# Queries and keys of the first head pair in two transfers each, and a scaling in two pieces

## The chip, the cores and the metric

The kernel runs on one core of a Trainium2 chip. The core's engines run their own instruction streams and meet at semaphores: TensorE (matrix products), VectorE, ScalarE, GpSimd, and SyncE (SP), which here only starts transfers. 16 DMA engines move data between DRAM and the on-chip memory; a transfer is started by an engine's queue, and it raises a semaphore by 16 when it has landed. The metric is the device time of one execution in microseconds, lower is better.

## What is computed

Block-causal attention over 4 x 8 heads of 576 positions and 64 columns, then a dense feed-forward layer, then a layer that sends each token to one of 8 experts:

```python
scores = scale * np.matmul(q, k.transpose(0, 1, 3, 2))      # (4, 8, 576, 64), scale = 1/8
scores = np.where(block_i >= block_j, scores, -1000000000.0)  # blocks of 64 positions
attn = np.exp(scores - np.max(scores, axis=-1, keepdims=True))
attn = attn / (np.sum(attn, axis=-1, keepdims=True) + 1e-09)
x = np.matmul(attn, v)                                       # then (2304, 512)
h = x @ w_in
x = np.maximum(0.01 * h, h) @ w_out                          # 512 -> 2048 -> 512
# tokens with x @ w_skip > 0: x + gate_w * (relu(x @ w1[e]) @ w2[e]), e the best of 8 experts
```

## The kernel before

The span has three stages: attention for 16 pairs of heads (with the first product of the dense layer filled in between, from pair 5 on), the rest of the dense layer, and the experts. Only the first microseconds of the first stage concern the change.

**A pair of heads** lies in tiles of 128 partitions, one head in each half: `q_sb[p % 2]` and `k_sb[p % 2]`, 576 columns of four bytes each, for pair p. The products of a pair are cut into nine units. Eight are query tiles of 128 rows, four per head, and query tile qt needs only the keys up to column 128 (qt + 1). The ninth, unit `TAIL` = 4, holds the last 64 query rows of both heads and needs all 576 columns of the keys. For the first six pairs TensorE computes the scores in five groups (`scores_of_both`, whose number is n): group 0 is query tile 0 of both heads (columns 0 to 127), group 1 is query tile 1 (queries 128 to 255, keys 0 to 255), group 2 is unit 4 (the last 64 queries, all keys), groups 3 and 4 are query tiles 2 and 3. Group 2 also needs room in the score buffers, that is two finished exponentials.

**Order.** Each engine's order is written out by hand in a loop over steps s, one unit each. VectorE first scales the queries by 1/8 (`scale_q`, L1118, waiting for queries and keys on `s_qk`), then takes each unit's row maximum (`maximum`, L1140, in step s for unit s), and copies transposed probabilities (L1146). ScalarE takes the exponential (L977) in step s once the maximum is there. TensorE runs groups 0 and 1 as soon as `s_q` says that the queries are scaled, then transposes the probabilities of unit 0 (L1491), then group 2 (L1435). The scaling of pair 1's queries is VectorE's in step 4.

**Loads at the start.** SP's queue starts the queries of pair 0 (`load_q(e, 0)`, L576), then queries and keys of pair 1, then a small weight tile; ScalarE's queue starts the keys of pair 0 (`load_k(e, 0)`, L581) and two transfers of values. Both queues feed the same 16 DMA engines. A tile of 128 rows of 2304 bytes goes as 128 packets. GpSimd meanwhile builds constants and masks (L763 to L800); its instructions L783 to L790 work on 4 x 512 mask tiles.

Of the kernel before, what the change touches and what calls it, by code (L numbers as in the profile page):

```python
# [11 lines left out]
ALU = mybir.AluOpType  # L12
# [3 lines left out]
P = 128  # L16
B, H, S, D = 4, 8, 576, 64
# [19 lines left out]
TAIL = 4  # L37
ROW_PAIRS = 6
ROW_UNITS = ROW_PAIRS * UNITS
FIRST_SPLIT = 2 * ROW_PAIRS  # L40


# [110 lines left out]
def by_act(p):  # L153

    return (7, 8) if p < ROW_PAIRS else (3, 8)
# [48 lines left out]
def build(nc, q_t, k_t, v_r, w_in, w_out, w_gs, w1, w2, out):  # L204
    ctx = ExitStack()
    with ctx:
        def sb(name, shape, dt=F32, scope=ctx):
            return scope.enter_context(nc.sbuf_tensor(name, shape, dt))
# [4 lines left out]
        def sem(name):  # L213
            return ctx.enter_context(nc.semaphore(name))
# [27 lines left out]
        q_sb = [sb(f"q_sb{i}", [P, S], F32, r2) for i in range(2)]  # L242
        k_sb = [sb(f"k_sb{i}", [P, S], F32, r2) for i in range(2)]
# [121 lines left out]
        s_wg = sem("s_wg")  # L365
        s_qk = [sem(f"s_qk{i}") for i in range(2)]
        s_v = [sem(f"s_v{i}") for i in range(2)]
        s_q = sem("s_q")
        s_mask = sem("s_mask")
        s_maskd = sem("s_maskd")  # L370
# [92 lines left out]
        def s_slot(u):  # L463
            p, i = divmod(u, UNITS)
            return 10 * p + i + (i > TAIL)

        def s_freed(u):

            last = s_slot(u) + (u % UNITS == TAIL) - S_RING
            if last < 0:  # L470
                return 0
            p, c = divmod(last, 10)
            return UNITS * p + c + 1 - (c > TAIL)
# [94 lines left out]
        def pair_in(x, p):  # L568

            b, h = p // KC, 2 * (p % KC)  # L570
            return x[b, h:h + 2, :, :].rearrange("h d s -> (h d) s")

        def load_q(e, p):
            if p >= 2:
                e.wait_ge(s_score, UNITS * (p - 1))
            e.dma_start(q_sb[p % 2][:, :], pair_in(q_t, p)).then_inc(s_qk[p % 2], 16)  # L576

        def load_k(e, p):
            if p >= 2:
                e.wait_ge(s_score, UNITS * (p - 1))  # L580
            e.dma_start(k_sb[p % 2][:, :], pair_in(k_t, p)).then_inc(s_qk[p % 2], 16)  # L581

        def load_head(e, n):

            p, odd = divmod(n, 2)
            b, h = p // KC, 2 * (p % KC) + odd
            if n >= FIRST_SPLIT + 2:
                e.wait_ge(s_qlo, n - FIRST_SPLIT - 1)
                e.wait_ge(s_klo, n - FIRST_SPLIT - 1)
            for half in (0, D):  # L590
                e.dma_start(k_raw[odd][half:half + D, :], k_t[b, h, :, :]).then_inc(s_head[odd], 16)
            cut = S - D
            to = QW - D if odd else cut
            for half in (0, D):
                if odd:
                    e.dma_start(q_raw[odd][half:half + D, 0:cut], q_t[b, h, :, 0:cut]).then_inc(s_head[odd], 16)
                    e.dma_start(q_raw[odd][half:half + D, to:QW], q_t[b, h, :, cut:S]).then_inc(s_head[odd], 16)
                else:
                    e.dma_start(q_raw[odd][half:half + D, 0:S], q_t[b, h, :, :]).then_inc(s_head[odd], 16)
# [12 lines left out]
        def _(e):  # L612
            def copy_k(n):
                e.wait_ge(s_khi, n - FIRST_SPLIT + 1)
                e.dma_start(k2[n % 2][0:D, :].bitcast(F32), k_st[n % 2][0:D, :].bitcast(F32)).then_inc(s_k2[n % 2], 16)
# [61 lines left out]
                    e.wait_ge(loaded, 16 * done)  # L677
                e.dma_start(dst, src).then_inc(loaded, 16)

            load_q(e, 0)  # L680
            load_q(e, 1)
            load_k(e, 1)
            e.dma_start(wg[:, :, :], w_gs).then_inc(s_wg, 16)
            for s in range(STEPS):
                p, i = divmod(s, UNITS)
# [74 lines left out]
        def _(e):  # L760
# [44 lines left out]
            def low_k(n):  # L805
                i, m = n % 2, n - FIRST_SPLIT
                e.wait_ge(*before[0])
                e.wait_ge(s_khi, m + 1)
                e.tensor_tensor(k_st[i][D:P, :], k_raw[i][D:P, :], k_st[i][D:P, :].bitcast(F32),
                                ALU.subtract).then_inc(s_klo, 1)  # L810
                before[0] = s_klo, m + 1
# [136 lines left out]
        def _(e):  # L948
            def high_q(n):
                odd, m = n % 2, n - FIRST_SPLIT  # L950
                e.wait_ge(s_head[odd], (96 if odd else 64) * (m // 2 + 1))
                if m < 2:
                    e.wait_ge(s_gap, N_GAP)
                else:
                    e.wait_ge(s_score, UNITS * (n // 2 - 1) + (UNITS if odd else TAIL + 1))
                e.activation(q_hi[odd][:, :], q_raw[odd][:, :], ACT.Copy, scale=D ** -0.5).then_inc(s_qhi, 1)
# [62 lines left out]
                for src, dst in pt_views(u):  # L1019
                    e.activation(dst, src, ACT.Copy).then_inc(s_pta, 1)  # L1020

            load_k(e, 0)
            load_v(e, 0)
            for s in range(STEPS):
                p, i = divmod(s, UNITS)
# [87 lines left out]

        @block.vector
        def _(e):
            def scale_q(p):
                e.wait_ge(s_qk[p % 2], 32 * (p // 2 + 1))
                e.tensor_scalar(q_sb[p % 2][:, :], q_sb[p % 2][:, :], D ** -0.5, None, ALU.mult).then_inc(s_q, 1)  # L1118
# [16 lines left out]
            def maximum(u):  # L1135
                src = score_out(u)
                e.wait_ge(s_score, u + 1)
                if u >= 4:
                    e.wait_ge(s_exp, u - 3)
                e.tensor_reduce(out=neg_max[:, u % 4:u % 4 + 1], in_=src, axis=AX.XY if u % UNITS == TAIL else AX.X,  # L1140
                                op=ALU.max, negate=True).then_inc(s_max, 1)
# [38 lines left out]
                e.tensor_tensor(g_lo[j % G_RING][:, :, :], g_raw[j % RAW_RING][:, :, :],  # L1180
                                g_hi[j % G_RING][:, :, :].bitcast(F32), ALU.subtract).then_inc(s_glo, 1)

            scale_q(0)
            for s in range(STEPS):
                p, i = divmod(s, UNITS)
                if s < N_UNITS:
                    maximum(s)
                if 3 <= s < N_UNITS + 3 and (s - 3) % UNITS not in by_act((s - 3) // UNITS):
                    copy_turned(s - 3)
                if i == 4 and p + 1 < ROW_PAIRS:  # L1190
                    scale_q(p + 1)
                if ROW_PAIRS <= p + 1 < N_PAIRS:
                    if i == 3:
                        high_k(2 * p + 2)
                    if i == 5:
                        low_q(2 * p + 2)
                    if i == 7:
                        high_k(2 * p + 3)
                if i == 0 and ROW_PAIRS <= p < N_PAIRS:
                    low_q(2 * p + 1)  # L1200
                if i == 0 and 1 <= p <= N_PAIRS:
                    invert(p - 1)
                if i == 2 and 1 <= p <= N_PAIRS:
                    copy_inverse(p - 1)
                if o_at(s):
                    copy_o(*o_at(s))
# [211 lines left out]
        def _(e):  # L1418
            def scores_of_both(n):

                p, d = divmod(n, GROUPS)
                u = UNITS * p + GROUP_LAST[d]
                if d == 0:
                    e.wait_ge(s_q, p + 1)
                if n == 0:
                    e.wait_ge(s_const, N_CONST)
                if s_freed(u):
                    e.wait_ge(s_exp, s_freed(u))
                c = 2 * BANK * (n % 2)
                q, k = q_sb[p % 2], k_sb[p % 2]  # L1430
                heads = (slice(0, D), slice(D, P))
                if GROUP_LAST[d] == TAIL:
                    for half in range(2):
                        for own in heads:
                            last = e.matmul(ps_s[own, c + BANK * half:c + BANK * half + S // 2], q[own, DM:S],  # L1435
                                            k[own, S // 2 * half:S // 2 * (half + 1)], start=True, stop=True)
                    last.then_inc(s_score, 1)
                    return
                qt = head_tile(u)[1]
                cols = P * (qt + 1)  # L1440
                for h, own in enumerate(heads):
                    e.matmul(ps_s[:, c + BANK * h:c + BANK * h + cols], q[own, P * qt:P * qt + P], k[own, 0:cols],  # L1442
                             start=True, stop=False)
                for h, own in enumerate(heads):
                    last = e.matmul(ps_s[:, c + BANK * h + cols - D:c + BANK * h + cols], mask_q[own, :], mask_k[own, :],  # L1445
                                    start=False, stop=True)
                last.then_inc(s_score, 2)

            def scores(u):

                p, i = divmod(u, UNITS)
                if i in (0, TAIL):
# [3 lines left out]
                    e.wait_ge(s_qlo, n - FIRST_SPLIT + 1)  # L1456
                if u == ROW_UNITS:
                    e.wait_ge(s_maskd, 32)
# [98 lines left out]
            for s in range(STEPS):  # L1557
                if ROW_UNITS <= s + 2 < N_UNITS:
                    scores(s + 2)
                if 2 <= s < N_UNITS + 2:  # L1560
                    transposes(s - 2)
                p, i = divmod(s, UNITS)
# [4 lines left out]
                if i in GROUP_AT:  # L1567
                    n = GROUPS * (p + (i > TAIL + 2)) + GROUP_AT[i]
# [228 lines left out]
```

## Time and profile before

| What | us |
|---|---|
| Median of 3 runs | 785.87 |
| The three runs | 784.16, 785.87, 787.03 |
| The profiled execution | 787.15 |
| its span, first to last instruction | 785.4 |
| TensorE busy | 761.7 |
| VectorE, ScalarE, GpSimd busy | 368.1, 303.3, 148.5 |

The page counts a busy engine from the first to the last moment of an instruction; its chain of waits leads back from the last instruction to what released it. "ACTq" and "SPq" are the queues that start transfers; times in the trace count from the span's start. A row with x2 stands for two instructions in a row.

### The profile page before, as it was taken

Reading aid. Unit: us, or ns where it says so; the run is one execution under the profiler, and the core shown is the slowest. Engines: PE = TensorE matmul, PEld = TensorE weight load, DVE = VectorE, ACT = ScalarE, POOL = GpSimd, SP = SyncE. Lnnn points to the kernel's source line nnn. Section 1 sums busy time; section 2 is a strip of 40 time slices with the busy share of each in tenths; the row PEclk is TensorE's granted clock in tenths of the full one; section 3 lists DMA queues with packets and bytes.
Section 4 is the critical chain, followed back from the end, with each engine's and each line's share of the span. In section 5 each row is a group of like instructions: output and inputs, shape, how many; then the busy total and the mean of one; then the engine's idle time right before and its main releaser. Section 6 shows DMA issues by size and latency. Waiting matters only on the chain.

```text
span 785.4 us, 13538 instructions
## 1 busy us (share of the span) xinstructions
PE 761.7 (97%) x4738; PEld 645.2 (82%) x4738; DVE 368.1 (47%) x771; ACT 303.3 (39%) x711; POOL 148.5 (19%) x193
## 2 busy tenths in 40 slices
PE   7999999999999998999999999999999999999997
PEld 3555888888888887999988888888878879999996
DVE  5667465533333554023355456465564342444644
ACT  4566565544344553234432223222121131333533
POOL 3226564221121331100020000000000031222222
PEclk9999999999999999999999999999999999999999
DMA  4334777554444541375666656556562037778730
GB/s 125 97 126 141 210 201 201 169 140 127 126 135 127 150 113 52 89 209 166 188 175 183 200 154 183 158 165 188 159 176 69 28 112 249 229 255 256 239 124 4
DMA packets 97671, 121.68 MB, mean 155 GB/s; under 512 B 14226, under 2 KB 60578, under 8 KB 97608
## 3 DMA queue, kind: packets, MB, share of 16 engines
q1 hardware_dynamic: 94776, 116.50, 50.6%
q0 software_dynamic: 2080, 3.77, 1.5%
q8 instruction: 36, 0.59, 0.3%
q10 hardware_dynamic: 752, 0.59, 0.2%
q14 instruction: 27, 0.22, 0.1%
HBM read 89.35 MB, written 31.57 MB: 154 GB/s over the span
## 4 chain that ended last, share of the span: by engine, by line
PE 91%; ACT 2%; issue 2%; DVE 1%; SPq 1%; DMA 1%; POOL 1%; DVEq 0%; POOLq 0%; ACTq 0%
PE ps_hid L1755 10%; PE ps_h L1535 9%; PE ps_x L1588 9%; PE ps_x L1590 8%; PE ps_x L1589 8%; PE ps_h L1537 8%; PE ps_h L1536 8%; PE ps_o L1517 6%; PE ps_t L1491 4%; PE ps_y L1767 3%; PE ps_y L1768 3%; PE ps_y L1766 3%; PE ps_s L1478 2%; PE ps_s L1442 1%; PE ps_s L1479 1%
## 5 line engine op out<-in xcount | busy, mean ns | idle before, releaser
L1535 PE MATMUL ps_h<-xh,win_h 128*128 128x384 f32 x384 | 136.4, 355 | 3.1 <-ACT act L989 2.4
L1537 PE MATMUL ps_h<-xh,win_l 128*128 128x384 f32 x384 | 128.7, 335 | 0.0
L1536 PE MATMUL ps_h<-xl,win_h 128*128 128x384 f32 x384 | 128.6, 335 | 0.0
L1588 PE MATMUL ps_x<-wout_h,g_hi 128*128 128x512 f32 x288 | 114.7, 398 | 0.0
L1590 PE MATMUL ps_x<-wout_h,g_lo 128*128 128x512 f32 x288 | 112.4, 390 | 0.0
L1589 PE MATMUL ps_x<-wout_l,g_hi 128*128 128x512 f32 x288 | 112.2, 389 | 0.0
L989 ACT ACTIVATE act<-ps_h 128x384 f32<-128x384 f32 x96 | 47.2, 492 | 155.7 <-PE ps_h L1537 155.7
L977 ACT ACTIVATE prob<-ps_s,neg_max 128x128 f32<-128x128 f32 (+3 forms) x144 | 78.8, 550 | 28.0 <-DVE neg_max L1140 27.4
L1146 DVE COPY pt<-ps_t 128x384 f32<-128x384 f32 (+4 forms) x113 | 48.4, 436 | 81.6 <-PE ps_t L1491 81.2
L1140 DVE TENSOR_REDUCE neg_max<-ps_s 128x1 f32<-128x128 f32 (+3 forms) x144 | 71.8, 504 | 30.4 <-PE ps_s L1445 15.2
L1755 PEld LDWEIGHTS ps_hid<-rows_t,w_sb 128*128 128x128 f32 x704 | 80.2, 192 | 1.7 <-issue 0.8
L1180 DVE TENSOR_TENSOR g_lo<-g_raw,g_hi 128x512 fp32r<-128x512 f32 x72 | 49.5, 688 | 67.2 <-ACT g_hi L999 66.8
L1755 PE MATMUL ps_hid<-rows_t,w_sb 128*128 128x128 f32 x704 | 80.5, 275 | 0.0
L1535 PEld LDWEIGHTS ps_h<-xh,win_h 128*128 128x128 f32 x384 | 72.1, 188 | 10.2 <-ACT act L989 5.1
L1536 PEld LDWEIGHTS ps_h<-xl,win_h 128*128 128x128 f32 x384 | 72.3, 188 | 0.0
L1537 PEld LDWEIGHTS ps_h<-xh,win_l 128*128 128x128 f32 x384 | 72.1, 188 | 0.0
L1588 PEld LDWEIGHTS ps_x<-wout_h,g_hi 128*128 128x128 f32 x288 | 54.1, 188 | 12.3 <-issue 2.0
L1590 PEld LDWEIGHTS ps_x<-wout_h,g_lo 128*128 128x128 f32 x288 | 54.1, 188 | 11.6
L1589 PEld LDWEIGHTS ps_x<-wout_l,g_hi 128*128 128x128 f32 x288 | 54.1, 188 | 10.4
L999 ACT ACTIVATE g_hi<-g_raw 128x512 fp32r<-128x512 f32 x72 | 43.8, 630 | 47.0 <-DVE g_raw L1175 31.1
L1491 PE MATMUL ps_t<-ident,prob 128*128 128x128 f32 x339 | 58.9, 278 | 1.4 <-issue 0.7
L1175 DVE SCALAR_TENSOR_TENSOR g_raw<-g_raw 128x512 f32<-128x512 f32 x72 | 49.2, 685 | 14.6 <-DMA g_raw<-hidden 14.3
(185 smaller groups left out, 1065.6 us busy)
## 6 DMA issues: line engine op xcount, KB each, us to landing
w_sb<-in_w SPq DMA_DIRECT2D x64, 512.0 KB, 5.3
hidden<-act SPq DMA_DIRECT2D x96, 192.0 KB, 2.3
g_raw<-hidden SPq DMA_DIRECT2D x72, 256.0 KB, 4.2
k_raw<-in_k_t SPq DMA_DIRECT2D x40, 144.0 KB, 3.0
x2rows<-x SPq DMA_DIRECT2D x18, 256.0 KB, 2.4
out<-x SPq DMA_DIRECT2D x18, 256.0 KB, 2.9
w_stage<-in_w_in SPq DMA_DIRECT2D x16, 256.0 KB, 3.1
w_stage<-in_w_out SPq DMA_DIRECT2D x16, 256.0 KB, 2.8
```

Source lines behind the costliest of these rows:

```text
L977: e.activation(prob_of(u), score_out(u), ACT.Exp, bias=neg_max[:, u % 4:u % 4 + 1], scale=1.0, accum_out=row_sum[p % 2][:, sum_column(u):s ...
L1140: e.tensor_reduce(out=neg_max[:, u % 4:u % 4 + 1], in_=src, axis=AX.XY if u % UNITS == TAIL else AX.X, op=ALU.max, negate=True).then_inc(s ...
L1175: e.scalar_tensor_tensor(out=raw[:, :, :], in0=raw[:, :, :], scalar=0.01, in1=raw[:, :, :], op0=ALU.mult, op1=ALU.max).then_inc(s_leaky, 1)
L1180: e.tensor_tensor(g_lo[j % G_RING][:, :, :], g_raw[j % RAW_RING][:, :, :], g_hi[j % G_RING][:, :, :].bitcast(F32), ALU.subtract).then_inc( ...
L1491: last = e.transpose(t_bank(u, P, P * kt, P * kt + P), tile[:, P * kt:P * kt + P], ident[:, :])
L1535: e.matmul(dst, win_h[:, f, kc, :], xh[slot][:, kc, :], start=kc == 0, stop=False)
L1536: e.matmul(dst, win_h[:, f, kc, :], xl[slot][:, kc, :], start=False, stop=False)
L1537: last = e.matmul(dst, win_l[:, f, kc, :], xh[slot][:, kc, :], start=False, stop=kc == KC - 1)
L1588: e.matmul(dst, hi, wout_h[:, f, :], start=f == 0, stop=False)
L1589: e.matmul(dst, hi, wout_l[:, f, :], start=False, stop=False)
L1590: last = e.matmul(dst, lo, wout_h[:, f, :], start=False, stop=f == FC - 1)
L1755: last = e.matmul(ps_hid[half][:, P * f - HALF * half:P * (f + 1) - HALF * half], w1_sb[i][:, c, P * f:P * f + P], rows_t[:, c, :], start= ...
```

## The change

Queries and keys of pair 0 come in two transfers each: columns 0 to 255 (`SOONER` = 256), counted on a new semaphore `s_sooner`, and columns 256 to 575, counted on `s_qk[0]` as before. SP issues both pieces of the queries, then pair 1 as before; ScalarE issues both pieces of the keys, then the values. VectorE scales columns 0 to 255 when the two first pieces are there, takes the maxima of units 0 and 1, and scales columns 256 to 575 in step 1, when the two second pieces are there. TensorE waits for the first scaling ahead of group 0 and for the second ahead of group 2. Counts of `s_q` for the later pairs are one higher. All else is as it was.

```diff
+SOONER = 2 * P
+        s_sooner = sem("s_sooner")
+        def load_sooner(e, sb_, x):
+            e.dma_start(sb_[:, 0:SOONER], pair_in(x, 0)[:, 0:SOONER]).then_inc(s_sooner, 16)
+            e.dma_start(sb_[:, SOONER:S], pair_in(x, 0)[:, SOONER:S]).then_inc(s_qk[0], 16)
...
-            load_q(e, 0)
+            load_sooner(e, q_sb[0], q_t)
             load_q(e, 1)
             load_k(e, 1)
...
-            load_k(e, 0)
+            load_sooner(e, k_sb[0], k_t)
             load_v(e, 0)
...
+            def scale_sooner():
+                e.wait_ge(s_sooner, 32)
+                e.tensor_scalar(q_sb[0][:, 0:SOONER], q_sb[0][:, 0:SOONER], D ** -0.5, None, ALU.mult).then_inc(s_q, 1)
+
+            def scale_rest():
+                e.wait_ge(s_qk[0], 32)
+                e.tensor_scalar(q_sb[0][:, SOONER:S], q_sb[0][:, SOONER:S], D ** -0.5, None, ALU.mult).then_inc(s_q, 1)
...
-            scale_q(0)
+            scale_sooner()
             for s in range(STEPS):
                 p, i = divmod(s, UNITS)
                 if s < N_UNITS:
                     maximum(s)
+                if s == 1:
+                    scale_rest()
...
-                if d == 0:
-                    e.wait_ge(s_q, p + 1)
                 if n == 0:
+                    e.wait_ge(s_q, 1)
                     e.wait_ge(s_const, N_CONST)
+                if n == 2:
+                    e.wait_ge(s_q, 2)
+                if p >= 1 and d == 0:
+                    e.wait_ge(s_q, p + 2)
```

VectorE at the start of the program, before; L1118 is the scaling, L1140 the maxima of units 0 to 3, L1146 a copy of transposed probabilities:

```order
L1118 TENSOR_SCALAR q_sb<-q_sb 128x576 [waits s_qk0]
L1140 TENSOR_REDUCE neg_max<-ps_s 128x1 [waits s_score] x4
L1146 COPY pt<-ps_t 128x128 [waits s_ptr]
L1140 TENSOR_REDUCE neg_max<-ps_s 128x1 [waits s_exp,s_score]
L1146 COPY pt<-ps_t 128x128 [waits s_ptr]
L1118 TENSOR_SCALAR q_sb<-q_sb 128x576 [waits s_qk1]
```

The same place of the changed program, whose lines are numbered anew (L1125 and L1129 are the two scalings of pair 0, L1155 the maxima, L1161 the copies):

```order
L1125 TENSOR_SCALAR q_sb<-q_sb 128x256 [waits s_sooner]
L1155 TENSOR_REDUCE neg_max<-ps_s 128x1 [waits s_score] x2
L1129 TENSOR_SCALAR q_sb<-q_sb 128x320 [waits s_qk0]
L1155 TENSOR_REDUCE neg_max<-ps_s 128x1 [waits s_score] x2
L1161 COPY pt<-ps_t 128x128 [waits s_ptr]
L1155 TENSOR_REDUCE neg_max<-ps_s 128x1 [waits s_exp,s_score]
L1161 COPY pt<-ps_t 128x128 [waits s_ptr]
L1133 TENSOR_SCALAR q_sb<-q_sb 128x576 [waits s_qk1]
```

One instruction has become two, the second of them behind two of the four maxima, with a wait of its own; nothing else has moved. On TensorE, the same stretch of the changed program (L1462 and L1465 groups 0 and 1 with their masks, L1511 transposes, L1455 group 2):

```order
L1462 MATMUL ps_s<-k_sb,q_sb 128x128 [waits s_const,s_q]
L1462 MATMUL ps_s<-k_sb,q_sb 128x128
L1465 MATMUL ps_s<-mask_k,mask_q 128x64 x2
L1462 MATMUL ps_s<-k_sb,q_sb 128x256 x2
L1465 MATMUL ps_s<-mask_k,mask_q 128x64 x2
L1511 MATMUL ps_t<-ident,prob 128x128 [waits s_exp]
L1455 MATMUL ps_s<-k_sb,q_sb 64x288 [waits s_exp,s_q]
L1455 MATMUL ps_s<-k_sb,q_sb 64x288 x3
```

The order is that of before; group 2 now waits for `s_q` beside `s_exp`.

## Rows read from the trace of the kernel before

**Rows 1.** The page: TensorE's busy time, and the chain by engine:
```profile
PE 761.7 (97%) x4738; PEld 645.2 (82%) x4738; DVE 368.1 (47%) x771; ACT 303.3 (39%) x711; POOL 148.5 (19%) x193
...
PE 91%; ACT 2%; issue 2%; DVE 1%; SPq 1%; DMA 1%; POOL 1%; DVEq 0%; POOLq 0%; ACTq 0%
```

**Rows 2.** The chain in order of time: start us, us, what:
```profile
0.81 3.78 DMA k_sb<-in_k_t
...
4.61 0.89 DVE q_sb L1118
...
5.55 0.80 PE ps_s L1442 x4
```

**Rows 3.** DMA packets, windows 1.8:2.8, 2.8:3.3, 3.3:3.8, 3.8:4.1 and 5:5.5:
```profile
q1 hardware_dynamic: 37, 0.09, 79.7%
q10 hardware_dynamic: 1, 0.00, 0.9%
...
q10 hardware_dynamic: 36, 0.08, 41.8%
...
DMA packets 90, 0.21 MB, mean 410 GB/s; under 512 B 1, under 2 KB 1, under 8 KB 90
...
q10 hardware_dynamic: 48, 0.11, 55.8%
...
q10 hardware_dynamic: 42, 0.09, 74.4%
...
DMA packets 337, 0.18 MB, mean 355 GB/s; under 512 B 4, under 2 KB 333, under 8 KB 337
```

**Rows 4.** VectorE's timeline: start us, us, instruction, idle before and its releaser:
```profile
4.61 0.88 DVE L1118 TENSOR_SCALAR q_sb<-q_sb 128x576 f32<-128x576 f32 x1 [4.61 <-DMA k_sb<-in_k_t]
6.44 0.49 DVE L1140 TENSOR_REDUCE neg_max<-ps_s 128x1 f32<-128x128 f32 x2 [0.95 <-PE ps_s L1445]
7.51 0.76 DVE L1140 TENSOR_REDUCE neg_max<-ps_s 128x1 f32<-128x256 f32 x2 [0.58 <-PE ps_s L1445]
...
10.04 0.76 DVE L1140 TENSOR_REDUCE neg_max<-ps_s 128x1 f32<-128x576 f32 x1 [1.58 <-PE ps_s L1435]
...
10.91 0.45 DVE L1118 TENSOR_SCALAR q_sb<-q_sb 128x576 f32<-128x576 f32 x1
...
16.85 0.27 DVE L1140 TENSOR_REDUCE neg_max<-ps_s 128x1 f32<-128x128 f32 x1
```

**Rows 5.** GpSimd's timeline, the mask instructions:
```profile
4.01 0.60 POOL L783 TENSOR_SCALAR_AFFINE_SELECT w_stage<-w_stage 4x512 f32<-4x512 f32 x1
4.58 0.60 POOL L785 TENSOR_SCALAR_AFFINE_SELECT w_stage<-w_stage 4x512 f32<-4x512 f32 x1
...
5.25 0.71 POOL L788 TENSOR_SCALAR_AFFINE_SELECT w_stage<-w_stage 4x512 f32<-4x512 f32 x1
...
5.92 0.60 POOL L790 TENSOR_SCALAR_AFFINE_SELECT w_stage<-w_stage 4x512 f32<-4x512 f32 x1
```

**Rows 6.** Timeline of ScalarE and TensorE around the start of group 2:
```profile
6.77 0.37 ACT L977 ACTIVATE prob<-ps_s,neg_max 128x128 f32<-128x128 f32 x1 [3.16 <-DVE neg_max L1140]
...
7.38 0.20 ACT L977 ACTIVATION_READ_ACCUMULATOR prob<-ps_s,neg_max 128x1 f32 x1
...
7.81 2.19 PE L1435 MATMUL ps_s<-k_sb,q_sb 64*64 64x288 f32 x8
```

**Rows 7.** From issue to landing, the keys of pair 1 (issued at 1.72):
```profile
DMA to landing us min/median/max: 5.6/5.6/5.6
```

**Rows 8.** Timeline of the issues of SP and of ScalarE's table load:
```profile
0.80 0.87 SPq L576 DMA_DIRECT2D q_sb<-in_q_t  x2
1.72 0.43 SPq L581 DMA_DIRECT2D k_sb<-in_k_t  x1
...
2.33 1.28 ACT L977 ACT_TABLE_LOAD   x1 [2.33 <-issue]
```

**Rows 9.** Waits in 60 to 95 us: us in total, times, longest:
```profile
PE ps_s L1468 <- DMA k<-k_st: 0.9, 1, 0.9
```

## The prediction

> **What bounds the kernel now.** I read the page's busy shares first: TensorE is busy in 97% of the span, and the chain that ended last runs through it for 91% [rows 1]. So nearly all of the span is matrix work that the change doesn't touch, and the time can only move where TensorE stands still. Next the chain in order of time [rows 2]. Its first link is the transfer of the keys of pair 0, 3.78 us from its issue at 0.81; then VectorE's scaling of the queries, 0.89; only at 5.55 does TensorE run its first instruction. These 5.5 us are all that the change can reach: 0.7% of the span. Everything behind them in the chain is started by a semaphore that the work before it raised, so an earlier start should shift the rest as a whole.
>
> **The sum's base.** The profiled execution took 787.15 us, of which 785.4 are the span and 1.75 lie around it. Terms are differences in this one execution; taken from its time they give the profiled time, taken from the median of the three runs, 785.87, the forecast. The profiled run is 1.28 us over that median, which is more than the effect I come to.
>
> **Part 1: the split transfers.** Before, q and k of pair 0 are 128 rows of 2304 bytes, a packet each, 8 packets for each of 16 DMA engines. From 1.8 to 2.8 us SP's queue (q1) moved 37 packets and ScalarE's (q10) one; from 2.8 both run side by side, and q10 has moved 1 + 36 + 48 + 42 = 127 packets by 4.1 [rows 3]. So the keys' 8 packets for each engine took 1.3 us from 2.8, turn about with SP's. The semaphore let VectorE go at 4.59 [rows 2], 0.49 after the last packet. One 2304-byte packet holds an engine 16 x 0.5 / 90 = 0.089 us (90 packets in half a microsecond), and 8 pairs of them should take 1.42, near the 1.3 seen. Packets of 512 bytes (mostly V's, 337 in half a microsecond) take 16 x 0.5 / 337 = 0.024 [rows 3]. On the line through these two, 1024 bytes take 0.042 and 1280 take 0.052. After the change, the first piece of k is 8 packets of 1024 bytes for each engine, turn about with SP's second piece of q (1280 bytes): 8 x (0.042 + 0.052) = 0.75, scaled by 1.3 / 1.42 to 0.69. That ends at 3.5, and with 0.49 behind it **the first pieces land at 4.0 instead of 4.59**. The start at 2.8 I leave as it is, since ScalarE's first issue stays where it was, at 0.81. Bounds: if SP's second piece didn't take turns, the 256 packets less the 38 already moved take 218 x 0.042 / 16 = 0.57, and landing is 3.85; if the pieces land only when all of q and k is through, it is 4.59 still, as the second issue on each queue and the doubled number of packets could make it. I take 4.0, which stays nearest to how the queues share the engines in the rows.
>
> The Trainium skill (DMA: Bandwidth & Descriptors, Anatomy of one DMA) speaks of a fixed part of about 2.0 us and a part by bytes at 436 GB/s, for another issue path. As an estimate from that page, the two pieces (262 KB) would land 0.75 us earlier than the two whole tiles (590 KB), where I have 0.6. The same page (Bandwidth) advises large transfers, which speaks against the split; if only that counted, the gain would be zero.
>
> **Part 2: the first scaling.** The row of the first scaling says 0.88 us, its twin for pair 1 at 10.91 says 0.45 for the same 576 columns [rows 4]. What differs is GpSimd: a mask instruction runs there from 4.58 to 5.18, another from 5.25 with 0.71 instead of its neighbours' 0.60 [rows 5], and by 10.91 GpSimd has nothing left. The first scaling ends 0.31 after 5.18, so it looks as if VectorE had waited for GpSimd's instruction. Cost of 256 columns: the maxima of 128 and 576 columns take 0.27 and 0.76 [rows 4], so 448 columns cost 0.49 and the fixed part is 0.13; of the scaling's 0.45 then 0.32 are columns, and 256 of them take 0.13 + 0.14 = 0.27, 320 of them 0.31. Arriving at 4.0, VectorE meets the mask instruction of 4.01 to 4.61. If it is held, it ends at 4.61 + 0.14 = 4.75; if not, at 4.27. If the extra 0.43 belongs to the first instruction, wherever it falls, it ends at 4.0 + 0.27 + 0.43 = 4.70. Two of three readings agree on 4.7, which I take. Before, it ended at 5.49, so **TensorE starts 0.8 us earlier**, at about 4.75.
>
> The Trainium skill (Advanced Engine Details and Errata, VectorE Performance Modes) says that VectorE's second SBUF port is shared with GpSimd and that the two block each other in two-port modes; by that rule the end is 4.75, without it 4.27. The 0.88 beside 0.45 agrees with it but doesn't prove it.
>
> **Part 3: the second scaling.** It stands on VectorE behind the second maximum and ahead of the third. Behind it wait that third maximum, and TensorE's block for the short tile, which needs all of q and k. Shifted by 0.8, the second maximum ends at 6.93 - 0.8 = 6.13 [rows 4]. GpSimd's last mask instruction runs from 5.92 to 6.52 [rows 5], so held, the scaling ends at 6.52 + 0.18 = 6.70; free, at 6.44. The third maximum would come at 7.51 - 0.8 = 6.71 and TensorE's block at 7.81 - 0.8 = 7.01, held by the second exponential (ended at 7.58) and its weight load [rows 6]. So **it costs nothing**, covered by the idle VectorE had there (0.58) and by TensorE's wait for ScalarE. Without that cover it would cost its 0.31. The data: q and k whole landed by 4.59; even the slowest of SP's first loads, the keys of pair 1, took 5.6 from issue [rows 7], and a second piece issued at 1.24 would by that land at 6.84.
>
> **Part 4: the queues.** One more issue on each of SP and ScalarE, 0.43 by the rows [rows 8]. On ScalarE it pushes V's loads and the table load, which would end at 3.61 + 0.45 = 4.06; the first exponential comes at 6.77 - 0.8 = 5.97 [rows 6, 8]. On SP it pushes pair 1, whose scaling comes at 10.91 - 0.8 and whose keys landed at 1.72 + 5.6 = 7.3. Both cost nothing. Later, from 70 to 84 us, the chain runs through SP's issues and TensorE waits 0.9 us for a copy of keys [rows 9]; what starts that stretch is progress too, so the shift should pass it. Sum: -0.6 (landing) - 0.2 (scaling) + 0 + 0 = -0.8; profiled 786.35, median **785.1**.
>
> **The rivals.**
> - *The scaling runs free of GpSimd.* For it: the row alone doesn't say why it took 0.88. TensorE starts at 4.3, gain 1.2: 784.7.
> - *Almost nothing.* The first pieces land after 4.61, since small packets and added issues eat the gain; the scaling meets the next mask instruction and ends at 5.18 + 0.14 = 5.32. Gain 0.2: 785.7. The same if the stretch at 70 to 84 us swallows the shift. For it: the slow 1.8 to 2.8, which fewer bytes may not shorten.
> - *Slower: the second pieces come late, and VectorE waits at the head of its queue.* TensorE's block now starts at 7.81; with 0.31 for the scaling this bites only if they land after 7.45. One microsecond behind the 6.84 above, at 7.84, it would start at about 8.2, 0.4 later than now: 786.3. Against it: the whole of q and k was through at 4.59, and nothing new stands ahead.
> - *The change does nothing of what it says* (the order is unchanged but for one VectorE instruction and two issues): 785.9, part of the second rival.
>
> **How the numbers follow.** Forecast 0.55, free scaling 0.2, almost nothing 0.2, slower 0.05. The cases lie between 784.7 and 786.3, and the landing's early bound (3.85) without a hold gives 784.5. But three runs of one kernel spread from 784.16 to 787.03, so a median of a few can be off by most of a microsecond either way: the range is 783.6 to 786.9. A change of 0.5%, about what a measurement of this kernel can tell from none, is 3.9 us. No case comes near; even an empty head of 5.5 us could hardly give it. Faster 0.02, same 0.96, slower 0.02.
>
> **What would show it.** In the profile after: VectorE's first scaling at about 4.0 instead of 4.61; its end near 4.7, or near 4.3 if GpSimd doesn't matter; TensorE's first row at 4.75; the second scaling between the second and third maximum with no wait on a transfer ahead of it; the block for the short tile near 7.0 instead of 7.81; the scaling of pair 1 near 10.1. A first scaling later than 4.4, or a block at 7.8 as before, would make the prediction wrong, and so would a span that differs by more than a microsecond with the head as said.

## Result: 0.15% faster, the head 1.4 us shorter

| | before | changed | |
|---|---|---|---|
| Median, 21 runs each | 785.98 | 784.49 | ratio 0.9985, 95% interval 0.9978 to 0.9992 |
| Span of the profiled execution | 785.4 | 784.6 | |
| Second comparison, 21 and 12 runs | 785.61 | 784.28 | ratio 0.9982, 0.9974 to 0.9991 |

The ratio is worth 1.2 us (0.6 to 1.7), the second 1.4 (0.7 to 2.0). The forecast was 785.1, 0.8 under before; the middle of each interval lies above that gain, and each interval contains it. Both are "no change" by the 0.5% bound of the prediction, although both intervals exclude 1: with this many runs a difference of 0.15% can be told from none.

The changed kernel's chain in order of time (start us, us, what), to be read beside [rows 2]:

```profile
0.81 2.91 DMA k_sb<-in_k_t
...
3.75 0.36 DVE q_sb L1125
...
4.15 0.80 PE ps_s L1462 x4
```

The keys' first piece landed 2.91 us from its issue instead of 3.78, the scaling took 0.36 instead of 0.89, and TensorE began at 4.15 instead of 5.55: 1.40 us earlier. VectorE's and GpSimd's timelines at the same place (start us, us, instruction), beside [rows 4, 5]:

```profile
3.75 0.35 DVE L1125 TENSOR_SCALAR q_sb<-q_sb 128x256 f32<-128x256 f32 x1 [3.75 <-DMA k_sb<-in_k_t]
5.04 0.49 DVE L1155 TENSOR_REDUCE neg_max<-ps_s 128x1 f32<-128x128 f32 x2 [0.94 <-PE ps_s L1465]
5.45 0.60 DVE L1129 TENSOR_SCALAR q_sb<-q_sb 128x320 f32<-128x320 f32 x1
6.11 0.76 DVE L1155 TENSOR_REDUCE neg_max<-ps_s 128x1 f32<-128x256 f32 x2
...
3.43 0.52 POOL L788 MEMSET w_stage<- 4x512 f32 x1
4.02 0.60 POOL L790 TENSOR_SCALAR_AFFINE_SELECT w_stage<-w_stage 4x512 f32<-4x512 f32 x1
...
5.26 0.60 POOL L795 TENSOR_SCALAR_AFFINE_SELECT w_stage<-w_stage 4x512 f32<-4x512 f32 x1
5.82 0.69 POOL L797 TENSOR_SCALAR_AFFINE_SELECT w_stage<-w_stage 4x512 f32<-4x512 f32 x1
```

The second scaling fills what was idle time of VectorE ahead of the third maximum, with no wait on a transfer. Group 2 stays 1.41 ahead (6.40 against 7.81). But the profiled span is only 0.8 shorter. The two traces against each other, by the start of each instruction:

| Milestone | before | changed | ahead by |
|---|---|---|---|
| TensorE's first product | 5.55 | 4.15 | 1.40 |
| Group 2 of pair 0 | 7.81 | 6.40 | 1.41 |
| Group 2 of pair 1 | 18.50 | 17.44 | 1.06 |
| Group 2 of pair 5 | 67.59 | 66.51 | 1.08 |
| SP issues pair 4's inverse sums | 75.60 | 74.80 | 0.80 |
| Span | 785.4 | 784.6 | 0.8 |

So 0.35 went between 9 and 11 us and 0.28 between 67 and 75. TensorE's timeline of the changed kernel, then that of before:

```profile
6.40 2.19 PE L1455 MATMUL ps_s<-k_sb,q_sb 64*64 64x288 f32 x8
8.52 0.47 PE L1511 MATMUL ps_t<-ident,prob 128*128 128x128 f32 x1
8.79 0.63 PE L1511 MATMUL ps_h<-ident,prob 128*128 128x128 f32 x2
9.35 1.65 PE L1462 MATMUL ps_s<-k_sb,q_sb 64*128 64x384 f32 x4
...
17.44 1.19 PE L1455 MATMUL ps_s<-k_sb,q_sb 64*64 64x288 f32 x8 [0.16 <-ACT prob L984]
```

```profile
10.75 1.33 PE L1442 MATMUL ps_s<-k_sb,q_sb 64*128 64x384 f32 x4
...
18.50 1.19 PE L1435 MATMUL ps_s<-k_sb,q_sb 64*64 64x288 f32 x8 [0.16 <-ACT prob L977]
```

The same eight rows of group 2 take 2.19 us in pair 0 and 1.19 in pair 1: TensorE's first products run at about half the later speed. That fits the lower of its two levels (1.2 and 2.4 GHz), but it is read from the lengths alone: the granted clock reads 1.00 in the window from 5 to 10 us of both kernels. Four rows of 64 x 384 take 1.65 when slow and 0.92 when fast (the experiments show that value); before, they took 1.33, so the rise came in their midst, after 0.92 (56% of the work at the slow pace), near 11.7. In the changed kernel they are slow to the end, near 11.0. The start moved by 1.40, the rise by 0.7 only: 0.7 us more at half speed, which is the lost 0.35. The prediction has no word on this.

The other 0.28 is in SP's issues ahead of the milestone at 75 us, where the chain runs through SP's queue. SP's timeline of the changed kernel, then of before:

```profile
72.60 1.52 SPq L604 DMA_DIRECT2D q_raw<-in_q_t  x1
74.16 0.60 SPq L622 DMA_DIRECT2D k<-k_st  x1
```

```profile
70.60 1.27 SPq L591 DMA_DIRECT2D k_raw<-in_k_t  x2
...
74.47 1.08 SPq L615 DMA_DIRECT2D k<-k_st  x1
```

Issues that take 0.60 elsewhere, or 1.11 for the pair, took 0.92 longer in one place after (1.52), and 0.16 and 0.48 longer in two places before: 0.28 more.

### The profile page after: what moved, and what is told of

It is laid out like the page before. It is cut to its first block, busy times and chain, and to the rows that moved or that the text cites. A ratio compares the mean times of both kernels' runs of the same rounds, so it can differ in the third digit from the quotient of the medians.

```text
span 784.6 us, 13542 instructions
## 1 busy us (share of the span) xinstructions
PE 761.9 (97%) x4738; PEld 645.2 (82%) x4738; DVE 368.8 (47%) x772; ACT 303.5 (39%) x711; POOL 148.6 (19%) x193
## 4 chain that ended last, share of the span: by engine, by line
PE 91%; ACT 2%; issue 2%; SPq 1%; DVE 1%; DMA 1%; POOL 1%; DVEq 0%; POOLq 0%; ACTq 0%
PE ps_hid L1775 10%; PE ps_h L1555 9%; PE ps_x L1608 9%; PE ps_x L1610 8%; PE ps_x L1609 8%; PE ps_h L1557 8%; PE ps_h L1556 8%; PE ps_o L1537 6%; PE ps_t L1511 4%; PE ps_y L1787 3%; PE ps_y L1788 3%; PE ps_y L1786 3%; PE ps_s L1462 2%; PE ps_s L1498 2%; PE ps_s L1499 1%
## 5 line engine op out<-in xcount | busy, mean ns | idle before, releaser
L1161 DVE COPY pt<-ps_t 128x384 f32<-128x384 f32 (+4 forms) x113 | 48.5, 437 | 81.4 <-PE ps_t L1511 81.0
L1155 DVE TENSOR_REDUCE neg_max<-ps_s 128x1 f32<-128x128 f32 (+3 forms) x144 | 72.0, 505 | 30.3 <-PE ps_s L1465 14.9
L1608 PEld LDWEIGHTS ps_x<-wout_h,g_hi 128*128 128x128 f32 x288 | 54.1, 188 | 12.3 <-issue 2.0
L1511 PE MATMUL ps_t<-ident,prob 128*128 128x128 f32 x339 | 58.9, 278 | 1.4 <-issue 0.7
```

The lines of the kernel that those rows point to most:

```text
L1511: last = e.transpose(t_bank(u, P, P * kt, P * kt + P), tile[:, P * kt:P * kt + P], ident[:, :])
L1608: e.matmul(dst, hi, wout_h[:, f, :], start=f == 0, stop=False)
```

## The experiments

Each kernel's edit is given against the changed kernel or the kernel before; L numbers of the traces are those of its own file.

### Each half alone

`transfers_alone`: split transfers, one scaling.

```diff
-                e.tensor_scalar(q_sb[0][:, 0:SOONER], q_sb[0][:, 0:SOONER], D ** -0.5, None, ALU.mult).then_inc(s_q, 1)
+                e.wait_ge(s_qk[0], 32)
+                e.tensor_scalar(q_sb[0][:, :], q_sb[0][:, :], D ** -0.5, None, ALU.mult).then_inc(s_q, 2)
...
-                if s == 1:
-                    scale_rest()
```

> The changed kernel with its split transfers, but VectorE waits for all four pieces and scales all 576 columns at once, ahead of the first maximum, as the kernel before does. If the doubled number of packets and the added issues cost something, the last piece lands later than the 4.59 of before; by the changed kernel's trace (second piece of the keys issued at 1.27, 3.3 to landing) it lands at about 4.6. So: scaling at 4.6, 0.88 long by the theory that it waits for GpSimd's mask instruction of 4.58 to 5.18, TensorE's start at 5.55 and the head as before to 0.1. The rival, that small packets slow the head, expects a landing of 4.8 or more.

The timelines of VectorE, GpSimd and TensorE:

```profile
4.54 0.46 DVE L1126 TENSOR_SCALAR q_sb<-q_sb 128x576 f32<-128x576 f32 x1 [4.54 <-DMA k_sb<-in_k_t]
...
4.58 0.89 POOL L792 TENSOR_SCALAR_AFFINE_SELECT w_stage<-w_stage 4x512 f32<-4x512 f32 x1
...
5.05 0.80 PE L1461 MATMUL ps_s<-k_sb,q_sb 64*128 64x128 f32 x4 [5.05 <-DVE q_sb L1126]
```

All four pieces were there at 4.54, against 4.59 to 4.73 for two whole transfers in the profiles: the doubled packets and the two added issues cost pair 0 nothing that this one trace shows. The expectation missed the length, and with it the head: it had 0.88 and a start at 5.55, and TensorE began at 5.05. VectorE began 0.04 ahead of GpSimd's mask instruction, took 0.46, and GpSimd's took 0.89 instead of 0.60. It isn't VectorE alone that waits: whoever begins second does. So these 0.50 hang on less than 0.1 us in the landing: at 4.61, in the kernel before, VectorE was the second.

`scaling_alone`: whole transfers, the scaling in two pieces.

```diff
-            load_sooner(e, q_sb[0], q_t)
+            load_q(e, 0)
...
-            load_sooner(e, k_sb[0], k_t)
+            load_k(e, 0)
...
-                e.wait_ge(s_sooner, 32)
+                e.wait_ge(s_qk[0], 32)
```

> Whole transfers as before, but VectorE scales 256 columns, takes two maxima and then scales 320. Landing 4.59 as before. By the theory that VectorE's scaling waits for GpSimd's running instruction (4.58 to 5.18), the first scaling ends at 5.18 + 0.14 = 5.32 and lasts 0.71, and TensorE starts at 5.37 instead of 5.55, a gain of 0.2. By the theory that the extra 0.43 belongs to whatever VectorE runs first, it lasts 0.70 too. By proportion (0.88 x 256 / 576) it lasts 0.39 and TensorE starts at 5.05.

```profile
4.64 0.69 DVE L1125 TENSOR_SCALAR q_sb<-q_sb 128x256 f32<-128x256 f32 x1 [4.64 <-DMA k_sb<-in_k_t]
...
6.68 0.32 DVE L1129 TENSOR_SCALAR q_sb<-q_sb 128x320 f32<-128x320 f32 x1
```

It ended at 5.33 (expected 5.32), and TensorE began at 5.38. The scaling in two pieces alone gives 0.17 of the 1.40. The second piece, at 6.68, came after the last mask instruction (which ended at 6.41) and took 0.32 (0.31 expected). The two halves alone gave 0.50 and 0.17 at the head, less than the 1.40 together: the hold makes the end of the scaling go in steps, by what GpSimd is doing when it begins. Both kernels had one run (785.36 and 785.46, before beside them 785.35), which says nothing of the time.

### GpSimd out of the way

`gpsimd_later_before` is the kernel before with one wait ahead of GpSimd's row fills; `gpsimd_later_after` the changed kernel with the same, against 2.

```diff
+            e.wait_ge(s_q, 1)
             e.memset(row_q, 1.0).then_inc(s_mask, 1)
```

> The kernel before, but GpSimd's two row fills and the mask instructions behind them wait until the queries are scaled. By the theory that the scaling waited for GpSimd, it lasts 0.45 instead of 0.88, and TensorE starts at 5.1 instead of 5.55. By the theory that VectorE's first instruction is slow by itself, it stays at 0.88.

> The changed kernel, but GpSimd's row fills and mask instructions wait until both scalings are done. By the same theory the first scaling lasts 0.27 instead of 0.35 and the second 0.31 instead of 0.60; TensorE starts 0.08 earlier and group 2 at most 0.1 earlier, since it waits for the exponential, not for the second scaling. By the rival both stay as they are. The time: within 0.3 us of the changed kernel.

VectorE and TensorE in the first, then in the second:

```profile
4.73 0.46 DVE L1119 TENSOR_SCALAR q_sb<-q_sb 128x576 f32<-128x576 f32 x1 [4.73 <-DMA k_sb<-in_k_t]
...
7.20 0.76 DVE L1141 TENSOR_REDUCE neg_max<-ps_s 128x1 f32<-128x256 f32 x2 [0.58 <-PE ps_s L1446]
...
5.25 0.80 PE L1443 MATMUL ps_s<-k_sb,q_sb 64*128 64x128 f32 x4 [5.25 <-DVE q_sb L1119]
```

```profile
3.59 0.29 DVE L1126 TENSOR_SCALAR q_sb<-q_sb 128x256 f32<-128x256 f32 x1 [3.59 <-DMA k_sb<-in_k_t]
...
5.24 0.32 DVE L1130 TENSOR_SCALAR q_sb<-q_sb 128x320 f32<-128x320 f32 x1
...
3.94 0.80 PE L1463 MATMUL ps_s<-k_sb,q_sb 64*128 64x128 f32 x4 [3.94 <-DVE q_sb L1126]
```

0.88 became 0.46, 0.35 became 0.29, 0.60 became 0.32. So the wait was for GpSimd, and "the first instruction is slow by itself" is out. TensorE began at 5.25 and at 3.94. As a gain over the changed kernel the last is 0.21 at the head, 0.16 of it because its pieces landed at 3.59 instead of 3.75. One run each (785.04 and 783.41) says no more about the time.

The row maxima aren't held in this way. The third and fourth took 0.76 here, from 7.20, while two mask instructions ran on GpSimd (6.87 to 8.14), and 0.76 in the kernel before, from 7.51, with GpSimd done at 7.47. They read the score buffers that TensorE writes, the scaling reads and writes `q_sb`.

### The size of the first pieces

`split_384`:

```diff
-SOONER = 2 * P
+SOONER = 3 * P
```

> The changed kernel with 384 columns in the first pieces instead of 256. By bytes alone, the landing lies on the line between 3.72 (256 columns) and 4.59 (all 576 in one): 3.72 + 0.87 x 128 / 320 = 4.07. By the theory that the slow stretch from 1.8 to 2.8 us belongs to packets of over 2 KB, the 1536-byte packets still escape it and the landing is near 3.9; by the theory that each queue's start is late by a fixed time, as in the prediction, it is 4.2 or more. The scaling then meets a GpSimd instruction at 4.02 to 4.62 and ends near 4.62 + 0.21 = 4.83.

```profile
4.08 0.75 DVE L1125 TENSOR_SCALAR q_sb<-q_sb 128x384 f32<-128x384 f32 x1 [4.08 <-DMA k_sb<-in_k_t]
```

Landing at 4.08 is nearest to the line by bytes (4.07). It is one run, and equal transfers landed up to 0.17 apart from trace to trace (VectorE began at 3.58 to 3.75 with 256 columns), so 3.9 and 4.2 aren't refuted by it. The scaling ended at 4.83, as worked out.

### The moment at which TensorE gets fast

`busy_first_after` lets TensorE work on zeros while it waits (VectorE clears the tile ahead of its scaling); `busy_first_before` does the same in the kernel before, ten times.

```diff
+            e.memset(prob[3][:, 0:P], 0.0).then_inc(s_busy, 1)
...
+            e.wait_ge(s_busy, 1)
+            for _ in range(7):
+                e.matmul(ps_o[:, 0:P], prob[3][:, 0:P], prob[3][:, 0:P], start=True, stop=True)
             scores_of_both(0)
```

> The changed kernel, but TensorE runs seven 128 x 128 products on a tile of zeros ahead of group 0, from about 1.1 to 4.1 us, while it would wait. In both profiles the first products run at about half the later speed (group 2's eight rows 2.19 us, the same eight for pair 1 1.19), and speed rises at about 11.7 before the change and 11.0 after it. Theory A, the rise follows TensorE's own activity: it now comes near 7 to 8 us, group 2 or what follows it gets shorter, pair 1's group 2 starts 1 to 2 us before the changed kernel's 17.44, and the time falls by 1 to 1.7 us against the changed kernel. Theory B, the rise comes at a fixed moment near 11: nothing changes, the head stays as in the changed kernel to 0.1.

> The kernel before with ten such products ahead of group 0, from about 1.1 to 5.4 us. Theory A: group 2 (at 7.81) still starts there, but runs in less than 2.19 us, speed has risen by 8, pair 1's group 2 starts 1.5 to 2 us before 18.50, and the time falls by 1.5 to 2 us: more than the change itself gains. Theory B: no difference.

TensorE in `busy_first_after`, where each of the seven products is two rows:

```profile
1.12 3.36 PE L1580 MATMUL ps_o<-prob 128*128 128x128 f32 x14 [1.12 <-DVE prob L1199]
4.41 0.80 PE L1464 MATMUL ps_s<-k_sb,q_sb 64*128 64x128 f32 x4
...
6.58 1.19 PE L1457 MATMUL ps_s<-k_sb,q_sb 64*64 64x288 f32 x8
...
8.18 0.92 PE L1464 MATMUL ps_s<-k_sb,q_sb 64*128 64x384 f32 x4
...
15.73 1.19 PE L1457 MATMUL ps_s<-k_sb,q_sb 64*64 64x288 f32 x8 [0.16 <-ACT prob L985]
```

and in `busy_first_before`, where the last of the products on zeros are fast already (20 rows in 4.15; 14 took 3.36):

```profile
1.12 4.15 PE L1560 MATMUL ps_o<-prob 128*128 128x128 f32 x20 [1.12 <-DVE prob L1184]
5.55 0.49 PE L1444 MATMUL ps_s<-k_sb,q_sb 64*128 64x128 f32 x4 [0.28 <-DVE q_sb L1119]
...
7.29 1.19 PE L1437 MATMUL ps_s<-k_sb,q_sb 64*64 64x288 f32 x8
```

Group 2 takes 1.19 in both, pair 1's group 2 starts at 15.73 and 16.44. The speed rose at about 6.5 and 4.6 us: theory B, a fixed moment near 11, is out.

| Kernel | median | before beside it | ratio (95%) |
|---|---|---|---|
| busy_first_after, 5 runs | 782.37 | 786.22 | 0.9954 (0.9940 to 0.9967) |
| busy_first_before, 8 runs | 783.65 | 786.22 | 0.9971 (0.9960 to 0.9981) |
| all_three, 5 runs | 782.62 | 786.22 | 0.9964 (0.9950 to 0.9978) |
| busy_six, 10 runs | 783.15 | 785.61 | 0.9969 (0.9958 to 0.9981) |
| busy_seven_again, 5 runs | 782.58 | 786.00 | 0.9961 (0.9948 to 0.9975) |

`all_three` adds GpSimd's wait to the seven products:

```diff
+            e.wait_ge(s_q, 2)
             e.memset(row_q, 1.0).then_inc(s_mask, 1)
```

> The changed kernel with the seven products ahead of group 0 and with GpSimd's row fills and masks behind the second scaling. Theory A expects the gain of the products alone plus at most 0.1, and the fastest kernel of the study, about 783; theory B the changed kernel's time less at most 0.1.

It came out no faster than the products alone (782.62 against 782.37, and the intervals overlap). The earlier scaling (3.64 to 3.93) found TensorE busy with zeros until 4.41, so the head gained nothing at its start.

`busy_six` has six products instead of seven:

```diff
-            for _ in range(7):
+            for _ in range(6):
```

> The changed kernel with six products on zeros ahead of group 0 instead of seven. Seven ended at about 4.4 where the scaled queries were there at 3.9 to 4.1; six end at 1.12 + 6 x 0.48 = 4.0. Group 0 starts at about 4.1, up to 0.3 earlier than with seven; the time is 782.4 less 0 to 0.3. If the earlier end of the products is lost again by a later rise, it is the same as with seven.

Group 0 began at 4.15 instead of 4.41, as expected, but in this execution the speed rose late:

```profile
6.40 2.19 PE L1457 MATMUL ps_s<-k_sb,q_sb 64*64 64x288 f32 x8
...
9.35 1.20 PE L1464 MATMUL ps_s<-k_sb,q_sb 64*128 64x384 f32 x4
```

The median, 783.15, missed the expected 782.1 to 782.4. Its interval overlaps that of seven; which is better stays open.

### The same kernels once more

`same_after` and `same_before` have no edit; `busy_seven_again` is `busy_first_after` again.

> The changed kernel once more, untouched, for the moment at which TensorE's speed rises. In the profiles so far it came between 3.5 and 6.9 us after TensorE's first product, in no order that goes with the edits. If the moment belongs to the kernel (theory K), it is 6.9 us after the first product again, at 11.0, and the 64 x 384 rows take 1.65 us again. If it is free of the program (theory F), it comes anywhere from 7.6 to 11.0, pair 1's group 2 starts where it may between 16.2 and 17.5, and the 0.33 us given back in the first comparison was that execution's, not the change's.

> The kernel before once more, untouched. Theory K: TensorE starts at 5.5 and its speed rises at 11.6, pair 1's group 2 starts at 18.50. Theory F: the rise comes anywhere from 9 to 12.4, that group starts between 17.4 and 18.9.

TensorE and VectorE in `same_after`:

```profile
3.65 0.45 DVE L1125 TENSOR_SCALAR q_sb<-q_sb 128x256 f32<-128x256 f32 x1 [3.65 <-DMA k_sb<-in_k_t]
...
6.40 2.16 PE L1455 MATMUL ps_s<-k_sb,q_sb 64*64 64x288 f32 x8
8.49 0.33 PE L1511 MATMUL ps_t<-ident,prob 128*128 128x128 f32 x1
...
8.97 0.92 PE L1462 MATMUL ps_s<-k_sb,q_sb 64*128 64x384 f32 x4
...
16.52 1.19 PE L1455 MATMUL ps_s<-k_sb,q_sb 64*64 64x288 f32 x8 [0.16 <-ACT prob L984]
```

Up to 8.4 TensorE's rows start within 0.01 us of those in the first profile of the changed kernel. Then the rise comes at 8.5 instead of 11.0, and pair 1's group 2 is 0.92 earlier (16.52 against 17.44). `same_before` went the other way: head as in the first profile (5.55, 7.80), rise at about 12.3, pair 1's group 2 at 18.81 instead of 18.50. So theory K is out: the moment isn't fixed by the kernel. It isn't free of what TensorE does either. Estimated from the rows that the rise cuts through, it came at 8.5 to 12.3 us in the nine profiles without products on zeros, and at 4.5, 4.6, 5.9, 6.5 and 10.0 in the five with them. After TensorE's first product it came between about 3.5 us (`busy_first_before`, `all_three`) and 8.9 us (`busy_six`).

> The changed kernel with seven products on zeros, untouched, once more. If the products bring the rise of TensorE's speed forward on the average, the median is again 782.0 to 782.9 and the ratio to before near 0.9955; if the first measurement was lucky in its moments, the median goes to that of the changed kernel, near 784. With six products the rise came 9.0 us after the first of them in the one profile, with seven 5.4, so the profile's own moment may be anything from 4.6 to 10.1.

The median is 782.58, in the range of the first reading: the gain of the products isn't luck. Its own profile has the rise at about 5.9.

The earlier rise is only about half of that gain. Pair 1's group 2 started at 15.7 in the three kernels with seven products, against 16.3 to 17.4 in the three profiles of nearly the same head without them (`after`, `same_after`, `gpsimd_later_after`). The rest came at SP's issues around 72 us. From pair 1's group 2 to SP's issue of pair 4's inverse sums passed 56.1 to 56.5 us in the five kernels with products and 56.9 to 57.5 in the nine without, each of which has one or two issues there that are together 0.4 to 1.0 us longer than elsewhere. SP in `gpsimd_later_after`, then in `busy_six`, which comes to the same place later and has none:

```profile
72.12 1.39 SPq L622 DMA_DIRECT2D k<-k_st  x1
```

```profile
72.77 0.59 SPq L623 DMA_DIRECT2D k<-k_st  x1
```

Why the kernels with products have no long issue there stays open; arriving earlier isn't the reason.

## Why the prediction was right, and where its sum was off

**What bounds, and what can be reached.** Right: the head of 5.55 us was all that moved, and the rest shifted behind it, though not as a whole (below). By its own signs TensorE was to start at 4.75, group 2 near 7.0 and pair 1's scaling near 10.1; they came at 4.15, 6.40 and 9.51, each 0.6 earlier than it said.

**Part 1, the landing, mis-sized.** Forecast 4.0, bounds 3.85 to 4.59; measured 3.72, outside the early bound (VectorE began at 3.75, and at 3.58 to 3.68 in the six other profiles with pieces of 256 columns). The landing, 0.87 earlier instead of 0.6, is the mis-sized term. The step that failed is "the start at 2.8 I leave as it is". The DMA queues of the changed kernel in 1.8 to 2.8 us (packets, MB, share); before they moved 37 and 1 packets [rows 3]:

```profile
q1 hardware_dynamic: 117, 0.11, 59.2%
q10 hardware_dynamic: 55, 0.06, 15.9%
```

With the issue at 0.81 in both, ScalarE's queue had moved 4 packets by 2.4 us and 19 more by 2.6, where it had moved one by 2.8 before. So its start wasn't a fixed time from the issue; it moved with the size of the packets on the two queues. What held it isn't shown: it wasn't a wait for all of SP's large packets, since only 37 of the 128 of its first tile had moved by 2.8. With 384 columns the landing lies near the straight line by bytes between 256 and 576 columns; a proportion would have done better than my count of packets in turns. The Trainium skill's advice of large transfers (DMA: Bandwidth & Descriptors, Bandwidth) would have had the split cost something; `transfers_alone` landed no later (4.54) than whole tiles (4.59 to 4.73).

**Part 2, the first scaling, right mechanism, wrong instruction.** The hold by GpSimd is shown by `gpsimd_later_before`, and by lengths that follow the arrival: starts at 3.58, 3.65, 3.67, 3.68 and 3.75 all ended at 4.08 to 4.10, that is 0.14 behind GpSimd's fill, which ends at 3.95 (3.43 + 0.52). I had VectorE arrive at 4.0, in the mask instruction; it came 0.25 sooner and met the fill ahead of it. Worked out with the right arrival, my own rule gives 3.95 + 0.14 = 4.09; measured 4.10. That makes 5.49 - 4.10 = 1.39 for the head instead of 0.8: 0.27 of the missing 0.6 are the landing, 0.33 the scaling, which gave 0.53 instead of 0.2. The first rival, the free scaling, has a time (784.7) nearer to the measured 784.49 than the forecast, for a wrong reason. The Trainium skill's sentence (Advanced Engine Details and Errata, VectorE Performance Modes), that the two engines block each other at the shared port, agrees with 0.88 against 0.46, and with GpSimd's 0.89 against 0.60 in `transfers_alone`. In `gpsimd_later_before` the same pair of engines never met.

**Part 3, the second scaling.** Right: it took 0.60, held until GpSimd's instruction of 5.26 to 5.86 was done (5.86 + 0.18 = 6.04, measured 6.05), and the third maximum and group 2 came where the shift alone puts them. Without the hold (`gpsimd_later_after`, 0.32) nothing more was gained there: its group 2 came 2.25 after TensorE's first product (3.94 to 6.19), as in the changed kernel (4.15 to 6.40).

**Part 4, the queues.** Right for the head: table load, V and pair 1 cost nothing; pair 1's scaling came at 9.51, 1.40 ahead. But the margin behind it shrank. Pair 1's keys, issued at 2.19, took 6.3 instead of 5.6:

```profile
k_sb<-in_k_t SPq DMA_DIRECT2D x1, 288.0 KB, 6.3
```

They landed at 8.5, where the prediction had 7.3, 1.0 ahead of the scaling instead of 3.6 (over all profiles with split transfers they landed at 7.3 to 8.6). "The shift should pass" the SP stretch at 70 us was not quite so: 1.08 went in and 0.80 came out in this pair of traces. One or two such long issues lie between 70.6 and 75.7 in all nine traces of kernels without products on zeros, and none in the five with them (above). What SP waits for there wasn't tried.

**What the sum lacked.** No row of the prediction spoke of TensorE's slow start, though 2.19 stands beside it in [rows 6]. It makes head time dearer and cheaper at once: work in it costs about double, and an earlier start isn't wholly kept. In the first comparison it took 0.35 of the gain, in the second profile of the changed kernel it gave 0.92 back. The forecast of 0.8 equals the profiled difference of 0.8 only because a head gain 0.6 too small met a loss of 0.63 that wasn't foreseen, which is luck. That the time came out inside the range, with a head 0.6 off, says little, since the range is 3.3 us wide.

The medians, 1.3 and 1.5 apart, with intervals from 0.6 to 2.0, suggest that on the average little of the 1.4 is lost, and can't settle it.

**The rivals.** "Almost nothing" failed with the landing; "slower" never came near, since the second pieces were there at 4.57 (the keys', 3.3 from issue at 1.27), ahead of the 5.45 at which VectorE came for them. "Does nothing of what it says" is refuted by the head.

## What to carry to other kernels

What stands ahead of the first product is read by the chain, and a split of the first transfer there was worth the bytes it left behind, since nothing that uses the rest came soon. Before costing an instruction of VectorE between tiles in on-chip memory, look at what GpSimd runs at that moment: here it ended when that one ended, plus its own columns. And where TensorE starts late, try to let it work on zeros while it waits: here that gave about 2 us, more than the change itself, and the two added up, though about half of it came at another place, for a reason that wasn't found.

## What the runs showed of the hardware

TensorE's first products ran at about half speed for 3.5 to 8.9 us, and the moment of the rise differed by 2.5 us between two executions of one and the same kernel (8.5 and 11.0), with the granted clock shown as 1.00 throughout. The Trainium skill (TensorE: Matmul & The Clock Gate, What's actually happening) says that what decides it runs free of the kernel, so that the moment varies, and gives ±500 ns; the runs agree that it varies, and show more.

The lower clock also came later, and there the granted clock shows it. Both first profiles have it near 312 us; the other twelve don't. The kernel before, then the same kernel once more (`same_before`), from 310 to 320 us (busy us and instructions by engine, granted clock, DMA share, GB/s):

```profile
310.00:320.00 10.00, 9.10 (x53) 7.11 (x54) 1.30 (x4) 1.17 (x3) 2.91 (x3) 0.83 0.16 51
```

```profile
310.00:320.00 10.00, 9.10 (x64) 7.81 (x63) 1.73 (x5) 2.10 (x5) 2.97 (x3) 1.00 0.23 71
```

In both TensorE stands still for 0.9 us in all, between 311 and 313. Behind that the granted clock of the first is 0.50, the lower level, from 312 to 315, and TensorE gets through 53 products in these 10 us instead of 64. It is the same kernel with the same pause, so the kernel doesn't fix whether the clock falls. From SP's issue of pair 4's inverse sums to the end passed 709.8 us in each of the two profiles with the fall, so it doesn't touch the difference of 0.8 between them, and 708.0 to 709.1 in the other twelve. With that, a late rise and a longer hold-up of SP, two profiles of the changed kernel have spans of 784.6 and 781.6: 3.0 us apart, twice what the change is worth. A gain of this size has to be read at its milestones and in medians, not in two spans.
